# A fused attention and two-stage expert kernel: the attention's last product with its values as stationary operand in two column groups, and SBUF transfers in place of partition-moving copies

## What is computed

```python
# attention: 2 batches x 8 heads, 768 rows, head size 64, all float32
q_bits = (q @ proj > 0); k_bits = (k @ proj > 0)        # 6 bits: a bucket for each row
mask = q_bucket[:, :, :, None] == k_bucket[:, :, None, :]
scores = np.where(mask, 0.125 * (q @ k.T), -1e9)
attn = np.exp(scores - scores.max(-1)); attn /= attn.sum(-1) + 1e-9
x = attn @ v                                            # heads side by side: 1536 x 512
# first dense stage: h = x @ w_in (2048 wide), a rational function of h, @ w_out
# second stage: each row goes to one of 8 experts (relu(x @ w1) @ w2), weighted
```

## Time and profile before

| | us |
|---|---|
| median of three runs | 897.37 (893.65 to 903.71) |
| profiled execution, its own time | 898.04 |
| its span, first to last instruction | 896.3 |
| TensorE busy (matmul) | 849.5 (95%) |
| VectorE busy | 749.2 (84%) |
| ScalarE busy | 606.5 (68%) |
| GpSimd busy | 336.3 (38%) |

### The profile page before, as it was taken

The page is one execution under the profiler, slowest core; times in us unless marked ns, Lnnn a source line. Parts: engine busy times, 40 slices in busy tenths (PEclk is TensorE's granted clock), DMA queues, the critical chain, the costliest instruction groups (busy, mean ns, idle before and its releaser), DMA issues.

```text
span 896.3 us, 17000 instructions
## 1 busy us (share of the span) xinstructions
PE 849.5 (95%) x5056; PEld 751.1 (84%) x5056; DVE 749.2 (84%) x1380; ACT 606.5 (68%) x1122; POOL 336.3 (38%) x289
## 2 busy tenths in 40 slices
PE   5999999999999999999999999999699999999996
PEld 3888889898888898889999999997587888888884
DVE  4689888888988868998877877886799999999982
ACT  1555656665565557887677766764289888898883
POOL 3353433435343501222222222221135766666452
PEclk9999999999999999999999999999889999999999
DMA  4111111211110102200000000003577111434940
GB/s 95 34 43 47 50 38 38 55 36 40 47 50 20 56 1 67 87 1 36 1 1 35 0 0 12 23 0 132 182 260 272 35 47 39 142 119 145 354 172 0
DMA packets 57473, 63.05 MB, mean 70 GB/s; under 512 B 29348, under 2 KB 39588, under 8 KB 57445
## 3 DMA queue, kind: packets, MB, share of 16 engines
q1 hardware_dynamic: 54404, 54.57, 19.2%
q0 software_dynamic: 3040, 8.13, 2.9%
HBM read 102.53 MB, written 8.13 MB: 123 GB/s over the span
## 4 chain that ended last, share of the span: by engine, by line
PE 80%; DVE 9%; issue 4%; ACT 2%; DMA 2%; POOL 1%; DVEq 0%; ACTq 0%; SPq 0%; POOLq 0%
PE ps_s L513 14%; PE ps_t L678 11%; PE ps_s L655 11%; PE ps_o L429 10%; PE ps_t L531 9%; PE ps_t L418 6%; PE ps_o L531 5%; PE ps_s L404 3%; PE ps_s L406 3%; DVE k_mask L918 2%; DVE row_max L932 2%; PE ps_s L664 2%; PE ps_p L393 2%; PE ps_p L380 1%; DMA xg<-mlp_out_scratch,idx_gather 1%
## 5 line engine op out<-in xcount | busy, mean ns | idle before, releaser
L1343 POOL TENSOR_TENSOR g_lo<-num_b,g_hi 128x384 fp32r<-128x384 f32 x64 | 65.7, 1026 | 245.4 <-ACT g_hi L798 162.9
L429 PEld LDWEIGHTS ps_o<-v_raw,probsT 128*128 128x128 f32 x1152 | 142.4, 193 | 6.0 <-issue 5.9
L429 PE MATMUL ps_o<-v_raw,probsT 128*128 128x64 f32 x1152 | 141.2, 273 | 0.2 <-ACT x_pair L733 0.2
L1226 DVE TENSOR_TENSOR w_lo<-w_raw,w_hi 128x1024 fp32r<-128x1024 f32 x76 | 124.6, 1695 | 3.5 <-ACT w_hi L849 1.6
L719 ACT ACTIVATE probs<-ps_s,exp_bias,exp_scale 128x768 f32<-128x768 f32 x96 | 94.9, 989 | 41.6 <-DVE exp_bias L942 41.4
L932 DVE TENSOR_REDUCE row_max<-ps_s 128x1 f32<-128x768 f32 x96 | 91.1, 949 | 16.1 <-PE ps_s L406 16.0
L733 ACT ACTIVATE x_pair<-ps_o,row_inv 128x64 f32<-128x64 f32 x96 | 30.2, 315 | 89.9 <-PE ps_o L429 89.9
L418 PE MATMUL ps_t<-ident,probs 128*128 128x128 f32 x576 | 82.4, 280 | 8.4 <-DVE probsT L947 6.2
L513 PE MATMUL ps_s<-xT_hi,win_hi 128*128 (+1 forms) x256 | 88.1, 344 | 0.0
L513 PE MATMUL ps_s<-xT_hi,win_lo 128*128 (+1 forms) x256 | 86.1, 336 | 0.0
L418 PEld LDWEIGHTS ps_t<-ident,probs 128*128 128x128 f32 x576 | 66.2, 146 | 23.6 <-issue 20.6
(11 more groups left out here) (210 smaller groups left out, 2247.1 us busy)
## 6 DMA issues: line engine op xcount, KB each, us to landing
w_raw<-in_moe_w_dram SPq DMA_DIRECT2D x152, 512.0 KB
win_raw<-in_moe_w_in_dram SPq DMA_DIRECT2D x16, 256.0 KB, 2.9
x_sb<-in_moe_w_out_dram SPq DMA_DIRECT2D x16, 256.0 KB, 2.8
qk_raw<-in_q_dram SPq DMA_DIRECT2D x16, 192.0 KB, 3.2
qk_raw<-in_k_dram SPq DMA_DIRECT2D x16, 192.0 KB, 3.4
v_raw<-in_v_dram SPq DMA_DIRECT2D x16, 192.0 KB, 2.4
mlp_out_scratch<-x_sb SPq DMA_DIRECT2D x12, 256.0 KB, 2.0
out_dram<-y_sb,idx_scatter POOLq DMA_INDIRECT x19, 2.9
```

The source lines that it names most:

```text
L429: mm = pe.matmul(ps_o[:, 0:D], probsT[slot][:, t, :], v_raw[par][:, t, :], start=(t == 0), stop=(t == QT - 1))
L1226: dve.tensor_tensor(w1_lo[par][:, c, :], w1_raw[:, c, :], w1_hi[par][:, c, :].bitcast(F32), ALU.subtract).then_inc(w1_lo_made, 1)
```

## The change

`attend` is turned round: the values (128x64) are stationary and the turned tile (128 columns) moves. Two tiles `c` and `c+1` are done together: tile `c` writes PSUM partitions 0 to 63 (column group 0 of the array), tile `c+1` partitions 64 to 127 (group 1), the two alternating. The work is cut in two parts of three blocks, one part in each step, so that each step has 12 records as before. The result comes out already turned: `turn_x`, `norm` and `x_pair` go. ScalarE copies 64+64 partitions x 384 of a head out of PSUM once (`evict_x`). The inverse row sums of a head (VectorE, 2 instructions of 6 columns in place of 12 of one) go through a DRAM scratch (`store_inverse`, `load_scale`) and come back as a row broadcast over the partitions; GpSimd multiplies (`scale_x`, operand read with a step of 6 elements), ScalarE and GpSimd split the product, and four transfers place it (`place_x`).

`move_hi` is gone: four SBUF to SBUF transfers a head (`place_hi`) move the pieces of `qkT_hi`, one of them in place of a GpSimd copy. `hash_qk` writes its two halves to the two column groups (64 columns each), one VectorE instruction makes all mask rows of a head, and four transfers place them (`place_masks`). SyncE's order is by head: `finish_head`, loads, `place_hi`, `place_masks`. TensorE's step is now: turn of `c-1`, part of an attend, scores of `c+2`; VectorE's: maximum of `c+1`, scale, bias, copy of `c-1`. At the passage ScalarE does `x_hi` of the last head within the first dense step and then waits for all of `place_x` before it rounds `w_out`; SyncE starts the loads of `w_out` after the last `place_x`; the last three attend parts stand between `mlp_up(0, 0)` to `mlp_up(0, 2)`. `split_win` rounds with a tensor-scalar instruction instead of a product with ones.

```diff
+            def place_hi(par):
+                hi = qkT_hi[:].bitcast(F32)
+                for target, rows, part in ((k_mask, slice(0, D), slice(D, P)), (q_mask, slice(0, D), slice(0, D)),
+                                           (k_cross, slice(0, D), slice(D, P)), (q_cross, slice(D, P), slice(0, D))):
+                    sp.dma_start(target[par][rows, :].bitcast(F32), hi[part, :]).then_inc(hi_in[par], 16)
+            def place_masks(par):
+                for hb in range(2):
+                    cols = slice(hb * HALF, (hb + 1) * HALF)
+                    for target, row in ((q_mask, HC * hb), (k_mask, HC * hb + ZK)):
+                        sp.dma_start(target[par][D:KR, cols].bitcast(F32),
+                                     mask_st[row:row + MR, :]).then_inc(mask_in[par], 16)
+            def place_x(i, par):
+                for parts, target in ((x_hi_st, xT_hi), (x_lo_st, xT_lo)):
+                    blocks = target[par * D:(par + 1) * D, :].bitcast(F32).rearrange(
+                        "p (q b g n) -> p q g b n", q=CD * NB, b=BLOCKS, g=2)
+                    where = bass.ds((i & (CD - 1)) * NB + ((i >> 2) & (NB - 1)), 1)
+                    for g in range(2):
+                        sp.dma_start(blocks[:, where, g, :, :], parts[par][g * D:(g + 1) * D, :].bitcast(F32).rearrange(
+                            "p (o b n) -> p o b n", o=1, b=BLOCKS)).then_inc(x_out[par], 16)
+            def store_inverse(par):
+                sp.dma_start(inv_dram[par].rearrange("(p j) -> p j", p=P),
+                             row_inv[:, par * QT:(par + 1) * QT]).then_inc(inv_out, 16)
+            def load_scale(par):
+                for g in range(2):
+                    sp.dma_start(scale_row[g * D:(g + 1) * D, 0:S - 1],
+                                 inv_dram[par:par + 1, g:g + S - 1].to_broadcast([D, S - 1])).then_inc(scale_in, 16)
...
+            def finish_head(i, par, placing=True):
+                m = 2 * i + par
+                hold(sp, inverted, m + 1)
+                store_inverse(par)
+                if placing:
+                    hold(sp, x_lo_made, START + m)
+                    place_x(i if par else i - 1, 1 - par)
+                    hold(sp, x_scaled, m)
+                hold(sp, inv_out, 16 * (m + 1))
+                load_scale(par)
+            def attention_head(i, par, first=False, more=True, more_qk=True):
+                m = 2 * i + par
+                if not (first and par == 0):
+                    finish_head(i if par else i - 1, 1 - par, placing=not first)
+                    if more or par == 0:
+                        hold(sp, attended, BLOCKS * m)
+                        load_v(m + 1, 1 - par)
+                if more and more_qk:
+                    hold(sp, qk_turned, 2 * m + 6)
+                    load_qk(m + 4, par)
+                if not (first and par == 0):
+                    hold(sp, win_lo_made, m)
+                if more or par == 0:
+                    load_win(m + 1, 1 - par)
+                if more:
+                    hold(sp, qk_hi_made, m + 3)
+                    hold(sp, scored, QT * (m + 1))
+                    place_hi(par)
+                    hold(sp, masked, m + 3)
+                    place_masks(par)
...
+            def hash_qk(i, par):
+                pe.wait_ge(qk_copied, 4 * i + 2 * par + 2)
+                for hb in range(2):
+                    mm = pe.matmul(ps_p[HC * hb:HC * (hb + 1), 0:HALF], hash_w[:],
+                                   qkT[:, hb * HALF:(hb + 1) * HALF], start=True, stop=True)
+                mm.then_inc(hashed, 1)
...
-            def attend(n, i, par, j, slot):
-                if j == 0:
-                    pe.wait_ge(v_in[par], 16 * (i + 1))
-                pe.wait_ge(pT_lo_half, n + 1)
-                pe.wait_ge(pT_hi_half, n + 1)
-                pe.wait_ge(normed, START + n)
-                for t in range(QT):
-                    mm = pe.matmul(ps_o[:, 0:D], probsT[slot][:, t, :], v_raw[par][:, t, :],
-                                   start=(t == 0), stop=(t == QT - 1))
-                mm.then_inc(attended, 1)
-            def turn_x(i, hb):
-                for t in range(TH):
-                    mm = pe.transpose(ps_p[:, t * P:(t + 1) * P], x_pair[:, hb * TH + t, :], ident[:])
-                mm.then_inc(x_turned, 1)
...
+            def attend(i, c, part):
+                n, par, b = STEPS * i + c, c // QT, (c % QT) // 2
+                if part == 0:
+                    pe.wait_ge(pT_lo_half, n + 2)
+                    pe.wait_ge(pT_hi_half, n + 2)
+                    if b == 0:
+                        pe.wait_ge(v_in[par], 16 * (i + 1))
+                        pe.wait_ge(x_raw_made, START + 2 * i + par)
+                for t in range(part * TH, (part + 1) * TH):
+                    for g in range(2):
+                        mm = pe.matmul(ps_o[g * D:(g + 1) * D, b * P:(b + 1) * P], v_raw[par][:, t, :],
+                                       probsT[(c + g) % 4][:, t, :], start=(t == 0), stop=(t == QT - 1))
+                if part == 1:
+                    mm.then_inc(attended, 1)
+            def step(i, c):
+                if there(i, c - 1):
+                    turn_probs(*at(i, c - 1), first=isinstance(i, int) and STEPS * i + c == 1)
+                part = (c + 1) % 2
+                if there(i, c - 3 - part):
+                    attend(*at(i, c - 3 - part), part)
+                if there(i, c + 2):
+                    scores(*at(i, c + 2))
+                if there(i + 1, 0):
+                    if c % QT in (0, 2):
+                        turn_qk(i + 1, c // QT, c % QT // 2)
+                    if c % QT == 4:
...
-            def norm(n, c):
-                par, j = c // QT, c % QT
-                act.wait_ge(attended, n + 1)
-                act.wait_ge(inverted, n + 1)
-                act.activation(x_pair[:, j, par * D:(par + 1) * D], ps_o[:, 0:D], ACT.Copy,
-                               scale=row_inv[:, c:c + 1]).then_inc(normed, 1)
-            def x_hi(i, hb):
-                act.wait_ge(x_turned, 2 * i + hb + 1)
-                act.activation(xT_hi[:, x_cols(i, hb)], ps_p[:, 0:HALF], ACT.Copy).then_inc(x_hi_made, 1)
...
+            def evict_x(i, par):
+                act.wait_ge(attended, BLOCKS * (2 * i + par + 1))
+                act.wait_ge(x_lo_made, START + 2 * i + par - 1)
+                act.activation(x_raw[par][:], ps_o[:, 0:HALF], ACT.Copy).then_inc(x_raw_made, 1)
+            def x_hi(i, par):
+                act.wait_ge(x_scaled, 2 * i + par + 1)
+                act.wait_ge(x_out[par], 16 * START + 64 * i)
+                act.activation(x_hi_st[par][:], x_raw[par][:], ACT.Copy).then_inc(x_hi_made, 1)
+            def step(i, c):
+                if there(i, c):
+                    exp_scores(i, c)
+                if there(i, c - 1):
+                    copy_probs(*at(i, c - 1))
+                if c % QT in (1, 3) and there(i + 1, 0):
+                    copy_qk(i + 1, c // QT, c % QT // 2)
+                done = (i, 0) if c >= QT else (i - 1, 1)
+                if c % QT == 2 and there(i, c - QT):
+                    evict_x(*done)
+                if c % QT == 5 and there(i, c - QT):
+                    x_hi(*done)
...
-            def move_hi(i, par, parts=(0, 1, 2)):
-                dve.wait_ge(qk_hi_made, 2 * i + par + 1)
-                hi = qkT_hi[:].bitcast(F32)
-                for part in parts:
-                    target, rows = ((q_cross[par][D:P, :], hi[0:D, :]), (k_mask[par][0:D, :], hi[D:P, :]),
-                                    (k_cross[par][0:D, :], hi[D:P, :]))[part]
-                    dve.tensor_copy(target, rows).then_inc(hi_moved, 1)
-            def mask_rows(i, par, hb, bank=ps_p):
-                cols = slice(hb * HALF, (hb + 1) * HALF)
-                dve.wait_ge(hashed, 4 * i + 2 * par + hb + 1)
-                dve.tensor_scalar(q_mask[par][D:KR, cols], bank[0:MR, 0:HALF], hash_thr[0:MR, 2:3], 1.0,
-                                  ALU.is_ge, ALU.mult)
-                dve.tensor_scalar(k_mask[par][D:KR, cols], bank[ZK:ZK + MR, 0:HALF], hash_thr[ZK:ZK + MR, 2:3], -BIG,
+            def mask_rows(i, par, first=False):
+                dve.wait_ge(hashed, 2 * i + par + 1)
+                if not (first and par == 0):
+                    dve.wait_ge(mask_in[1 - par], 64 * (i + par))
+                dve.tensor_scalar(mask_st[:], ps_p[:, 0:HALF], hash_thr[:, 2:3], hash_thr[:, 3:4],
                                   ALU.is_ge, ALU.mult).then_inc(masked, 1)
...
+            def invert_sums(i, par):
+                m = 2 * i + par
+                cols = slice(QT * par, QT * (par + 1))
+                dve.wait_ge(exped, QT * (m + 1))
+                dve.tensor_scalar(sum_eps[:, cols], row_sum[:, cols], 1e-9, None, ALU.add).then_inc(summed, 1)
+                dve.wait_ge(summed, m + 1)
+                if not (isinstance(i, int) and i == 0):
```

(64 more changed lines are left out.)

419 lines of the change are left out of this document (173 added, 246 removed).

## The result

The changed kernel takes 865.22 us (median, 863.61 to 867.38), beside 898.62 for the kernel before on the same chips; the ratio is 0.963, with a 95% interval of 0.957 to 0.969. The forecast was 862, in a range of 843 to 918. The profiled execution has a span of 861.9 in place of 896.3, so 34.4 us are to be found.

What follows compares the result with a forecast made beforehand. TensorE, busy for 95% of the span, was taken to bound the kernel. The terms -25.0 - 8.3 - 5.1 - 11.6 + 6.6 + 7.8 + 0 = -35.6 took 898.0 to 862 us, range 843 to 918.

Steps and rivals of the forecast that it cites:

- part 1: Attend turned round, two column groups side by side: 1.02 in place of 1.28 a step, 25.0 us less.
- 7 slots of 0.107: Attend's 12 records of a step, second group starting one slot after the first: 7 slots, 0.75 us.
- part 2: A head's hash in two column groups: 3 slots and one narrow-operand switch, 1.23 us; 8.3 us less.
- part 3: TensorE's `turn_x` transposes go: 16 x 0.32, 5.1 us less.
- The switch: Going to a narrow stationary operand and back on TensorE: 0.27 us, once a step in attend (bounds 0 and 0.54).
- part 4: TensorE's waits for VectorE's moving copies, 11.6 us, go; 6.6 us of waits kept (bounds 0 and 13).
- VectorE's loop: Scores, maximum, scale and bias, copy, hand-over, TensorE's step: 4.7 us for two steps of 4.8, covered; half the waits kept.
- part 5: SyncE's issues, 11 us of a head's 16, and the DRAM round cost nothing while hidden; hidden with little left.
- One sign that I had named as absent: In the steady part, no wait of ScalarE for GpSimd that ends in TensorE; no size given.
- rival B: DRAM round late for ScalarE's `x_hi` in step 5, exponentials and TensorE behind: 2 us over gives about 894; chance 10%.
- part 6: From last scores to first `mlp_down`: last head's result, transfers and `w_out` in a row, 7.8 us later (bounds 3 and 12).
- part 7: At the start, first scores wait for transfers instead of copies, VectorE's later copies go: 0 us (bounds -4 and +4).

Runs made afterwards that it cites:

- experiments 1 and 2: Changed kernel, attend's records group by group instead of alternating: 878.88 us; changed kernel, all attend records in one column group, half of x wrong: 915.56 us.
- experiment 7: Changed kernel with earlier scale loads, passage edit and last attends ahead of `mlp_up`, plus both attend parts in one step of two: 849.73 us.
- experiment 8: Kernel before, with only VectorE's three moving copies a head made SBUF to SBUF transfers on SyncE: 885.67 us beside 897.79.
- experiments 3 and 4: Changed kernel, scale-row loads issued after two of four `place_x` transfers: 854.64 us; changed kernel, DRAM round of the row sums left out: 853.29 us.
- experiment 9: Changed kernel with SyncE's start order altered: small constants before head 1's q and k, heads 2 and 3's q and k earlier: 856.54 us.

## Why the prediction came out right, step by step

The total was right (862 for 865.2), and so was the mechanism. The terms were off by more than the total, in both directions.

**Attend (part 1).** Forecast 2.40 a tile, measured 2.37: 27.8 less in place of 25.0. Right in what decides, that everything hangs on the second column group, and that it works: experiments 1 and 2. Mis-sized inside: I counted 7 slots of 0.107, since I let the second group start a slot after the first; the two start 0.006 us apart, and there are 6.

**Hash (part 2).** For the same reason (two slots in place of three) 0.88 in place of my 1.23: 13.2 less in place of 8.3. A hash of four records still costs what one of two did.

**`turn_x` (part 3)**, 5.1, went as said: its instructions are gone, and no row contradicts the size; it wasn't tried alone.

**The switch** of 0.27, read from one hash, holds: 0.29 in experiment 7.

**Waits (part 4).** Right that the copies' waits go (experiment 8), though they were 9 and not 11.6: the sum had TensorE's own work of a pair 0.35 too small. Wrong in what takes their place. I kept 6.6 for VectorE's loop. There are 9.0, all of them for exponentials that stand behind `x_hi`, and the chain there runs through SyncE. The loop of 4.7 us is real, but it lies just under TensorE's pace, as worked out, and shows only when TensorE gets faster (experiment 7). So the change gains nearly nothing in waits (9.2 before, 9.0 after), where 5.0 were forecast.

**Transfers (part 5).** This is the step that failed: "They cost nothing while hidden", on the ground of two sums, the time that a head gives to each chain and SyncE's issues (11 us of 16; about 12 measured). Each fits within a head. What I didn't draw is that they close into a ring: the load of the scale row starts GpSimd's work, that work releases `place_hi` and `place_masks`, and the next load stands behind these in the same queue. The ring takes 16.7 a head beside TensorE's 15.8, and sets the pace, once the slack is used up, although no member is busy all the time. One sign that I had named as absent is there, ScalarE's wait for GpSimd that ends in TensorE. That is rival B's end (ScalarE late in `x_hi`), but not the cause that B gave, the load on the DMA engines and small descriptors, since reordering one queue cures it (experiments 3 and 4). It costs 10.6, of which 8.7 show at the last scores.

**Passage (part 6).** Forecast 7.8 later, measured 10.2, the chain as described. (The terms as written come to 25.7 behind the last scores and so to 7.3 later; 7.8 is a slip.) From `evict_x` of the last head to the rounding of `w_out` it takes 9.3, as forecast (9.1). But `evict_x` itself comes 13.4 behind the last scores and not 10.8, and 1.6 of this is TensorE's first `mlp_up` waiting for GpSimd's last `split_win`, which I had not looked at.

**Start (part 7).** I took 0. The first scores came 5 us late and another wait of 6.5 followed. Up to the first scores of pair 1 the change gained 1.5, where the forecast's terms for one pair give 3.7 (25.0 / 8 for the attends and 0.6 for `turn_x`): 2.2 worse, within the bounds of 4. There was more to be had here, 8.7 us by the order of the loads alone (experiment 9).

So the forecast hit its number partly by luck: 7.6 us better in TensorE's own work from pair 1 on, 5 worse in waits, 2.4 worse in the passage, 2.2 worse at the start, and 0.6 better in what follows, 1.2 worse in all (34.4 in place of 35.6).

## What to carry to other kernels

When transfers take over work from an engine, write down every queue as a ring for one period: what the first issue releases, and which later issue in the same queue waits for that. Sums of busy time don't show it, and neither does a look at the first periods: a ring that is 0.9 us longer than TensorE's work used up its slack first and cost nothing for the first heads. Moving the one issue that feeds the ring ahead of those that nobody waits for was worth a third of the change here. Here a stationary operand of 64 columns paid only with a second product in the other half of the array, and most with the records of the two alternating; and the first and last periods of such a pipeline want their own look at the order of loads and at which tiles lie over which.

## What the runs showed of the hardware that I had not expected

- Two column groups stream fully side by side for float32 records: a record each 0.055 us with alternating groups, 0.114 in one group, 0.079 with six of one and then six of the other. In the last case the second stream begins 0.28 us after the first, behind its third record (experiment 1).
- Issuing a transfer on SyncE takes 0.71 to 0.87 us for 12 partitions x 1.5 KB (18 KB), as against medians of 0.35 for 192 KB of v and 0.61 for 192 KB of q.
- Two of VectorE's tiny instructions for the hash constants took 1.8 and 1.5 us beside GpSimd's remainders at the start of the changed kernel, and ended with them (at 10.18 and 12.03 us, GpSimd's at 10.14 and 12.02); others beside them took 0.14 to 0.16. With the constants loaded earlier the same two took 0.17 and 0.15 (experiment 9). Why these two are held is not shown.
